# Two per-row-scalar multiplies in place of one broadcast multiply in an attention step on GpSimd

## The reference

```python
# q, k, v: (4, 8, 576, 64)
scores = q @ k.T / sqrt(64)                   # per batch and head
scores = where(0 <= i - j < 128, scores - slope[h] * |i - j|, -1e9)
attn = exp(scores - max(scores))
attn = attn / (sum(attn) + 1e-9)              # <- the step that is touched
x = (attn @ v) as (2304, 512)
# mixture 1, 4 experts: x = sum_e p[:, e] * (relu(x @ w1[e]) @ w2[e]),  w1[e]: 512 x 1024
# mixture 2: logits = x @ phi (32 slots), softmax over rows, 8 experts of 4 slots,
#            softmax over slots, back to (2304, 512)
```

## Time and profile before

| | before |
|---|---|
| median of 3 runs | 998.73 us (997.78 to 1002.35) |
| the profiled execution | 997.73 us, its span 995.9 us |
| TensorE matmul busy | 957.9 us (96% of the span) |
| VectorE, ScalarE, GpSimd busy | 596.0, 446.6, 659.6 us |
| mean granted TensorE clock | 0.982 |

### The profile page before, as it was taken

The page is one execution under the profiler, slowest core; times in us unless marked ns, Lnnn a source line. Parts: engine busy times, 40 slices in busy tenths (PEclk is TensorE's granted clock), DMA queues, the critical chain, the costliest instruction groups (busy, mean ns, idle before and its releaser), DMA issues.

```text
span 995.9 us, 18516 instructions
## 1 busy us (share of the span) xinstructions
PE 957.9 (96%) x6067; PEld 793.7 (80%) x6067; DVE 596.0 (60%) x1175; ACT 446.6 (45%) x943; POOL 659.6 (66%) x587
## 2 busy tenths in 40 slices
PE   8879999999999989999999999989999999999896
PEld 6558888888888878888888888878888899887532
DVE  5895556565565776556566565665655656556602
ACT  4774444444444544444444444634434344432312
POOL 5988676667669796666667668797866676661000
PEclk8799999999999989999999999999999999999998
DMA  8633314214214213314214212119212122137896
GB/s 251 187 92 114 107 43 128 91 42 130 88 48 126 89 43 112 109 43 127 92 42 130 88 46 82 43 50 333 73 56 84 42 84 69 58 104 283 348 377 238
DMA packets 86403, 116.90 MB, mean 117 GB/s; under 512 B 6208, under 2 KB 56896, under 8 KB 86352
## 3 DMA queue, kind: packets, MB, share of 16 engines
q1 hardware_dynamic: 84736, 109.89, 33.9%
q0 software_dynamic: 1616, 6.36, 1.7%
HBM read 111.51 MB, written 4.72 MB: 117 GB/s over the span
## 4 chain that ended last, share of the span: by engine, by line
PE 82%; POOL 7%; DVE 4%; issue 4%; DMA 1%; ACT 1%; DVEq 0%; SPq 0%; POOLq 0%; ACTq 0%
PE banks L1364 36%; PE banks L1346 32%; PE banks L1304 3%; PE banks L1256 2%; POOL h_lo L665 2%; PE banks L1497 1%; PE banks L1524 1%; PE banks L1278 1%; POOL ws_lo L656 1%; PE banks L1280 1%; DVE w_lo L1043 1%; POOL w_lo L656 1%; PE banks L1237 1%; DMA out<-slot_w 1%; PE banks L1423 1%
## 5 line engine op out<-in xcount | busy, mean ns | idle before, releaser
L1071 DVE SCALAR_TENSOR_TENSOR acc<-banks,prob,acc 128x512 f32<-128x512 f32 x288 | 215.5, 748 | 191.4 <-PE banks L1364 191.2
L1364 PE MATMUL banks<-w_hi,h_hi 128*128 128x512 f32 x576 | 227.1, 394 | 5.0 <-POOL h_lo L665 2.7
L1364 PE MATMUL banks<-w_hi,h_lo 128*128 128x512 f32 x576 | 229.2, 398 | 0.0
L1364 PE MATMUL banks<-w_lo,h_hi 128*128 128x512 f32 x576 | 228.4, 396 | 0.0
L665 POOL TENSOR_TENSOR h_lo<-c,h_hi 128x384 fp32r<-128x384 f32 x144 | 149.8, 1057 | 103.4 <-ACT c L842 103.2
L840 ACT ACTIVATE h_hi<-c 128x384 fp32r<-128x384 f32 x144 | 75.0, 521 | 169.5 <-PE banks L1364 100.6
L656 POOL TENSOR_TENSOR ws_lo<-w_sum,ws_hi 128x1024 fp32r<-128x1024 f32 x48 | 117.0, 2438 | 33.4 <-ACT ws_hi L816 33.4
L1346 PE MATMUL banks<-xT_hi,ws_hi 128*128 128x384 f32 x384 | 131.3, 342 | 3.1 <-POOL ws_lo L656 3.1
L1346 PE MATMUL banks<-xT_lo,ws_hi 128*128 128x384 f32 x384 | 129.1, 336 | 0.0
L1346 PE MATMUL banks<-xT_hi,ws_lo 128*128 128x384 f32 x384 | 128.8, 335 | 0.0
L1364 PEld LDWEIGHTS banks<-w_hi,h_hi 128*128 128x128 f32 x576 | 108.7, 189 | 23.9 <-issue 9.2
(11 more groups left out here) (169 smaller groups left out, 1612.5 us busy)
## 6 DMA issues: line engine op xcount, KB each, us to landing
w_raw<-w SPq DMA_DIRECT2D x96, 512.0 KB, 4.1
slot_w<-m2w SPq DMA_DIRECT2D x4, 2048.0 KB, 11.9
v_b<-v_n SPq DMA_DIRECT2D x24, 256.0 KB, 5.4
slot_early<-m2w POOLq DMA_DIRECT2D x3, 2048.0 KB, 12.5
slot_early<-m2w SPq DMA_DIRECT2D x3, 2048.0 KB, 12.3
v_a<-v_n SPq DMA_DIRECT2D x20, 256.0 KB, 5.3
out<-slot_w SPq DMA_DIRECT2D x9, 512.0 KB, 4.7
q_b<-q_t SPq DMA_DIRECT2D x12, 288.0 KB, 4.6
```

Of the source, the lines that this page charges most:

```text
L1071: dve.scalar_tensor_tensor(acc[:, tile, :], ps_y[tt % 2][:, :], prob[:, tile, bass.ds(e, 1)], acc[:, tile, :], ALU.mult, ALU.add).then_inc ...
L1364: ins = pe.matmul(ps_y[tt % 2][:, :], hh[:, f, tt * P:(tt + 1) * P], wp[u % 2][:, f, :], start=m == 0, stop=m == 3 * FT - 1)
```

## The change

`norm` did both heads with one `tensor_tensor`: the tile of 128 x 2 x w (w is 192, or 128 for a first tile) times the reciprocals, which are read as an operand of the same shape by repeating each value w times. Now it is two `tensor_scalar` instructions, one for each head, over 128 x w each, with the reciprocal of the row as a scalar operand of one value for each partition. Only the second signals `s_norm`. In the loop (not in the lead) an empty instruction stands ahead of the two. Nothing else is touched.

```diff
                 w = width(p, a)
                 buf = pr_of(n, a, lead)
                 pool.wait_ge(s_rinv, place(n, a) + 1)
-                pool.tensor_tensor(buf[:, :, 0:w], buf[:, :, 0:w],
-                                   rinv[:, a, :].unsqueeze(2).broadcast_to([P, 2, w]),
-                                   ALU.mult).then_inc(s_norm, 1)
+                if not lead:
+                    pool.nop(nofuse=True)
+                for h in range(2):
+                    ins = pool.tensor_scalar(buf[:, h, 0:w], buf[:, h, 0:w], rinv[:, a, h:h + 1], None, ALU.mult)
+                ins.then_inc(s_norm, 1)
```

## The result

The changed kernel takes 1009.43 us (median of 4 runs, 1009.33 to 1009.85) against 999.18 us before (median of 4, 997.78 to 1002.35). The ratio is 1.0109, with a 95% interval of 1.009 to 1.0129: 10 to 11 us slower, where 1.4 us less were forecast and 1002.5 us was the upper end of the range. The profiled execution has a span of 1007.5 us against 995.9.

What follows compares the result with a forecast made beforehand. TensorE was taken to bound the loop, and GpSimd to be nearly always busy in the lead (37 of 40 us). Lead terms of 0.55, 0.4, 0.2 and 0.2 us, loop zero, made 1.4 us less: 997.3 us, range 993.5 to 1002.5.

Steps and rivals of the forecast that it cites:

- the price of the new instruction: Each norm on GpSimd: two scalar multiplies take 0.72 us a pair at 192 columns, against 0.83 for the old instruction.
- The upper end: Highest bound for a scalar multiply on GpSimd: the form with two full operands, 0.60 us at 192 columns, 1.15 a pair.
- the term of 0.11 us less for each norm: GpSimd in the lead: each wide norm 0.11 us shorter; five on the chain give 0.55 us less.
- Its line: GpSimd's queue in the lead: rival 1 decides from 1.12 us a pair (0.58 us an instruction) upwards.
- five norms on the chain and a third of the others: Lead: five chain norms give 0.55 us less; the other 12 in the busy stretch, counted a third, 0.4 us less.
- the 17 from 30 us on: Lead, 30 to 67 us: rival 1 has these 17 norms become the bound, 17 x 0.33 = 5.6 us more.
- rival 1: GpSimd's queue, 30 to 67 us: scalar form dear, 1.15 us a pair, 5.6 us more, 1004.3 us; chance 0.12.
- The covers: Loop: 2 us between norm and transposes, 1.3 at the change of pass, hide the pair and empty instruction; no change.
- the change of pass: Loop: order of VectorE's L1023 and GpSimd's work may shift; counted zero, 2 us either way in the range.
- The mean of VectorE's L1023 in the lead: Lead: falls, as L1023 waits for half a norm only; two such waits on the chain give 0.2 us less.
- Rival 3: Lead, 53 to 68 us: VectorE instructions slip between the halves, up to 2.8 us more, 999 to 1001 us; chance 0.24.

Runs made afterwards that it cites:

- The probe: Kernel before with a row of GpSimd multiplies and copies behind its last instruction: scalar 2.5 ns a column, full operand 2.1; no ratio given.
- memsets: Kernel before with a memset of 320 spare columns on GpSimd ahead of each of the 27 norms of the lead: ratio 1.0053.
- the constant: Kernel before with one scalar multiply by 1.0 over both heads for each norm of the lead, normalisation left out there: ratio 1.0028.
- half the norm: Kernel before with the norms of the lead multiplying the first head only, by a broadcast operand: ratio 0.998.

## Why the prediction was wrong

**The step that failed is the price of the new instruction.** The prediction took it from the nearest row in kind, an instruction of GpSimd with one stream in and one out (0.35 us at 192 columns), and went a quarter of the way up to the broadcast form, for 0.39 us (0.72 us a pair with the overlap). It measured 0.75 to 0.78. The upper end failed too: it was the form with two full operands, 0.60 us, on the thought that a form that reads less can't be dearer for a column than one that reads more. The probe shows 2.5 ns a column against 2.1. The rule of the Trainium skill that the prediction set beside it, that GpSimd is near line rate with one input (GPSIMD Engine Reference, section 4.1), holds here for the copy, 0.9 ns a column, and not for the multiply with a scalar or a constant. So the pair cost 1.50 us, not 0.72, and the term of 0.11 us less for each norm was 0.70 us more.

**The place was right.** Of the rivals it was the first, the dear scalar form, which got a chance of 0.12: GpSimd's queue in the lead becomes the bound with all that stands between the norms. It was given 1004.3 us, because its pair was capped at 1.15 us, the same bound that failed. Its line, that it decides (0.5% slower) from 1.12 us a pair, is neither borne out nor refuted: about 0.32 us more for each norm measured 1.0053 with memsets, but 0.35 us with the constant 1.0028, below the line.

**The weight in the lead.** That five norms on the chain and a third of the others count fits a gain: at half the norm, 2 us less. (The others in the busy stretch are 13, not twelve, since the one at 14.3 us lies outside it; that is 0.04 us.) It was wrong as a rule for a loss, since a longer queue puts nearly all 27 on the chain. I had counted the 17 from 30 us on for it; those of 12 to 29 us had idle time between them (4.5 of the 6.0 us from the first to the last), and 0.70 us each used it up, so that the chain stays on GpSimd from the first norm. With the measured price rival 1's own sum, 12 wide and 5 narrow norms, would have come to 11.4 us, close to what was measured, but by luck: what holds is 27 norms, 18.1 us, less 6.0 us of idle time and 1.4 us of the rest.

**The loop.** The covers were right: 1.3 to 2 us between a norm and its transposes hide 0.70 us more and the empty instruction, and the kernel with the new form in the loop alone shows no change (0.9963 to 1.0004). Nothing moved at the change of pass beyond the scatter either: what lies behind the lead took 922.0 us against 922.1, among profiles from 921.6 to 924.0.

**The rest.** The mean of VectorE's L1023 in the lead was to fall, since it would wait for half a norm only. It rose: the 27 of them took 12.9 us against 10.6, with a median of 272 ns against 299 but a longest of 2.5 us against 0.9. That sign failed; it is nothing beside the queue. Rival 3 had as its sign a gap between the halves. There is none: in all 27 norms of the lead the second half starts 0.01 to 0.03 us before the end of the first. What happens is that a half lasts longer, in three norms (the second half of the one at 47.63 us takes 1.39 us where 0.77 is usual). It is one of the four halves merged in this row, which take 2.99 us where nothing disturbs them:

```profile
46.15 3.61 POOL L634 TENSOR_SCALAR pr<-pr,rinv 128x192 f32<-128x192 f32 x4
```

Together these three lengthen GpSimd's queue by 1.2 us. The norms of the kernel before lasted 1.6 us longer in all than undisturbed ones, so rival 3 adds nothing. GpSimd's busy time in 30 to 70 us, which was to fall to 35.3 us, is 39.7. The mean granted clock of TensorE in 50 to 70 us is 0.73 where it was 1.00, so part of that stretch is at 1.2 GHz now, with TensorE waiting for norms in between. I take it as a consequence, since GpSimd and not TensorE fills the chain there; no run isolates it.

## What to carry to other kernels

An instruction that no row of the trace shows has no upper bound from its relatives: here the form that reads one stream took 2.5 ns a column and those that read two took 1.67 and 2.1. Where the whole sign hangs on such a price, widen the range to two or three times the nearest row, and time a few of it at the tail of the kernel, where the engine is idle, before rewriting anything. And an engine that is busy for 37 of 40 us in one stage is lopsided: making its work shorter gained little (2 us for 8.4 us less queue), making it longer cost a third at first and nearly all of it once its idle time was used up.

## What the runs showed of the hardware

On GpSimd a multiply in float32 with one scalar for each row takes 0.27 us and 2.5 ns a column, with a constant 0.18 us and 2.5 ns, with a value that is read as a broadcast operand 0.16 us and 1.67 ns, and with a full operand 0.16 us and 2.1 ns. I had expected the opposite order. The broadcast form is the cheapest of them at every width tried (64, 128, 192 and 384 columns; the full operand was tried at 128 and 192 only). These are single rows of one execution at the tail of a kernel; the kernels themselves show 0.78 us for the scalar at 192 columns, 1.18 us for the constant at 384 and 0.53 us for the broadcast at 192, which agree.
